# Loading the second weight strip of a fused attention and mixture kernel in eight 128 KB pieces over units 6 to 13, with its split on GpSimd in units 14 and 15

## The reference

```
scores = scale * q @ k^T           # 4 x 8 heads, 576 positions, head width 64
mask: 0 <= i - j < 64
attn = softmax(masked scores)      # then attn @ v -> x, 2304 tokens x 512
xn = x / sqrt(mean(x*x) + 1e-6) * rms_g
x  = silu(xn @ w_gate) * (xn @ w_val) @ w_out        # width 1536
e  = argmax(x @ moe2_w_gate)                         # 8 experts
out[token] = softmax(x @ moe2_w_gate)[e] * (relu(x @ w1[e]) @ w2[e])
```

## Time and profile before

| quantity | value |
|---|---|
| median of three runs | 817.53 us |
| profiled execution | 815.81 us |
| its span, first to last instruction | 814.0 us |
| TensorE (PE) busy | 802.3 us, 99% |
| VectorE (DVE) busy | 489.3 us, 60% |
| ScalarE (ACT) busy | 304.8 us, 37% |
| GpSimd (POOL) busy | 204.6 us, 25% |
| granted TensorE clock | 0.999 of full |

### The profile page before, as it was taken

One profiled execution on the slowest core, in us unless ns is written; L12 is line 12 of the kernel. 1 busy time (PEld: TensorE's weight loads), 2 busy tenths in 40 slices (PEclk: granted clock), 3 DMA queues, 4 the chain that ended last, 5 costly groups with the idle time before them and its releaser, 6 DMA issues.

```text
span 814.0 us, 15142 instructions
## 1 busy us (share of the span) xinstructions
PE 802.3 (99%) x4785; PEld 724.8 (89%) x4786; DVE 489.3 (60%) x999; ACT 304.8 (37%) x666; POOL 204.6 (25%) x183
## 2 busy tenths in 40 slices
PE   7999999999999999999999999999999999999996
PEld 7999999999999999999999999998888888888885
DVE  7888645667657764857586677727226445564252
ACT  7988742121321132131213124334324534543341
POOL 4596596031004000400220000052920110110100
PEclk9999999999999999999999999999999999999999
DMA  7997960020002002000200012226353643655100
GB/s 218 297 333 259 329 245 1 0 79 1 1 1 79 0 1 76 4 1 1 78 0 1 1 43 100 104 79 221 128 181 130 246 151 131 256 189 193 54 15 26
DMA packets 39809, 86.57 MB, mean 106 GB/s; under 512 B 4094, under 2 KB 13566, under 8 KB 39232
## 3 DMA queue, kind: packets, MB, share of 16 engines
q1 hardware_dynamic: 35568, 75.41, 26.9%
q0 software_dynamic: 3360, 10.23, 3.5%
q10 hardware_dynamic: 816, 0.12, 0.1%
HBM read 72.37 MB, written 14.16 MB: 106 GB/s over the span
## 4 chain that ended last, share of the span: by engine, by line
PE 96%; DMA 2%; issue 1%; SPq 0%; DVE 0%; ACT 0%; POOL 0%; POOLq 0%; ACTq 0%; DVEq 0%
PE ps L1085 28%; PE ps L1084 28%; PE ps L1083 28%; PE ps L1018 3%; PE ps L1230 2%; PE ps L1053 2%; PE ps L1038 1%; PE ps L1150 1%; PE ps L1012 1%; DMA vt<-vW 1%; DMA kt<-kT 0%; DMA qraw<-qT 0%; PE ps L1260 0%; DMA out<-osb,sidx 0%; PE ps L1268 0%
## 5 line engine op out<-in xcount | busy, mean ns | idle before, releaser
L1083 PE MATMUL ps<-xn_hi,GV_hi 128*128 128x384 f32 x576 | 194.1, 337 | 0.0
L1085 PE MATMUL ps<-xn_hi,GV_lo 128*128 128x384 f32 x576 | 193.3, 336 | 0.0
L1084 PE MATMUL ps<-xn_lo,GV_hi 128*128 128x384 f32 x576 | 192.9, 335 | 0.0
L1083 PEld LDWEIGHTS ps<-xn_hi,GV_hi 128*128 128x128 f32 x576 | 108.2, 188 | 2.8
L1084 PEld LDWEIGHTS ps<-xn_lo,GV_hi 128*128 128x128 f32 x576 | 108.2, 188 | 2.7
L1085 PEld LDWEIGHTS ps<-xn_hi,GV_lo 128*128 128x128 f32 x576 | 108.1, 188 | 0.0
L826 ACT ACTIVATE h_hi<-ps 128x384 fp32r<-128x384 f32 x72 | 35.5, 493 | 163.1 <-DVE ps L1446 161.4
L1476 DVE CUSTOM_DVE_ANT_0 ps<-ysb,wrb 128x512 f32<-128x512 f32 x120 | 92.3, 770 | 6.0 <-ACT ysb L833 1.0
L820 ACT ACTIVATE sig<-ps 128x384 f32<-128x384 f32 x71 | 35.0, 493 | 159.3 <-PE ps L1085 140.1
L1085 PE MATMUL ps<-Wo_hi,h_lo 128*128 128x512 f32 x216 | 85.5, 396 | 0.0
L1084 PE MATMUL ps<-Wo_lo,h_hi 128*128 128x512 f32 x216 | 85.3, 395 | 0.0
(11 more groups left out here) (183 smaller groups left out, 1407.9 us busy)
## 6 DMA issues: line engine op xcount, KB each, us to landing
EW_raw<-w SPq DMA_DIRECT2D x32, 1024.0 KB, 5.8
vt<-vW SPq DMA_DIRECT2D x16, 512.0 KB, 5.2
y_rows<-ysb SPq DMA_DIRECT2D x6, 768.0 KB, 4.1
kt<-kT SPq DMA_DIRECT2D x47, 96.0 KB, 4.6
qraw<-qT SPq DMA_DIRECT2D x15, 288.0 KB, 3.9
xraw<-xT_rows SPq DMA_DIRECT2D x5, 768.0 KB, 5.6
xT_rows<-xo SPq DMA_DIRECT2D x12, 288.0 KB, 3.6
raw_out<-w_out SPq DMA_DIRECT2D x3, 1024.0 KB, 7.9
```

The costliest lines, as they stand in the source:

```text
L1083: nc.tensor.matmul(out, a_hi, b_hi, start=start, stop=False)
L1084: nc.tensor.matmul(out, a_hi, b_lo, start=False, stop=False)
L1085: return nc.tensor.matmul(out, a_lo, b_hi, start=False, stop=stop)
```

## The change

Strip 0 is loaded as before, in units 2 to 5. The halves of strip 1 are each cut into two quarters of 128 KB (the rows of one of the two 128-row tiles in a half, 1 KB a partition), and one quarter is loaded in each of the units 6 to 13, gate in even, value in odd units. It stands in SyncE's queue at the place where the half stood. SyncE's two loops become unrolled code. GpSimd splits strip 1 after n = 14 and 15, and scales the first rows after n = 13.

```
-EARLY_HALVES = 4
+QUARTERS = 4
...
-            return 16 * (min(2 * c + 2, EARLY_HALVES) + max(c + 1 - EARLY_HALVES // 2, 0)) + 16
+            return 16 * ((2, 2 + QUARTERS)[min(c, 1)] + max(c - 1, 0)) + 16
...
-                sp.dma_start(GV_raw[:, bass.ds(h, 1), kind, :, :].rearrange("p a k f -> p (a k f)"),
-                             (w_gate, w_val)[kind][bass.ds(h, 1)].rearrange("a p f -> p (a f)")).then_inc(w_in[kind], 16)
+                sp.dma_start(GV_raw[:, h, kind, :, :].rearrange("p k f -> p (k f)"),
+                             (w_gate, w_val)[kind][h]).then_inc(w_in[kind], 16)
+
+            def load_quarter(i, kind):
+
+                h, k = 2 + i // 2, i % 2
+                sp.wait_ge(w_in[kind], 16 * (2 + i) + 16)
+                sp.dma_start(GV_raw[:, h, kind, k, :],
+                             (w_gate, w_val)[kind][h, :, k * STRIP:(k + 1) * STRIP]).then_inc(w_in[kind], 16)
...
+                if quarter is not None:
+                    load_quarter(quarter, u)
...
-            with sp.Fori(KEPT + 1, EARLY_HALVES + 1) as pair:
+            for i in range(QUARTERS - 1):
                 for u in range(2):
-                    unit(2 * pair + u, u, half=pair - 1)
-            with sp.Fori(EARLY_HALVES + 1, UNITS // 2 - 2) as pair:
-                for u in range(2):
-                    unit(2 * pair + u, u)
+                    unit(2 * (KEPT + 1 + i) + u, u, quarter=i)
             for u in range(2):
-                unit(UNITS - 4 + u, u, q=u == 0)
+                unit(UNITS - 4 + u, u, q=u == 0, quarter=QUARTERS - 1)
...
-            strip_at = {7: 0, 8: 1, 11: 2, 12: 3}
+            strip_at = {7: 0, 8: 1, 14: 2, 15: 3}
             square_at = {9: (0, 1), 10: (2, 3)}
-            scale_at = {14: range(KD)}
+            scale_at = {13: range(KD)}
```

More of the change, by code:

```diff
@@ L440, in _, with unit @@
             load_keys(3, 1)
-            def unit(n, u, q=True, k=True, half=None, store=store_xT):
+            def unit(n, u, q=True, k=True, half=None, quarter=None, store=store_xT):
                 store(n - 2, u)
```

## The result

The changed kernel takes 818.82 us, the median of 22 runs (816.04 to 820.87), against 817.31 us for the kernel before (22 runs, 815.63 to 818.71). The ratio is 1.002, interval 1.0011 to 1.0028: slower by 0.9 to 2.3 us; 0.2%, which I had set as the bound between no change and slower, is 1.64 us and lies within it. A second set of runs gave 1.0023 (1.0012 to 1.0033). The forecast was 818.6 us. Its closeness is partly luck: it was a change of +1.03 us on top of 817.53, the median of three runs, and the measured changes are +1.51 us on top of 817.31 and, in the second set, +1.79 on top of 817.36.

The account below looks back on a forecast made before the run. TensorE was taken as the bound, busy 802.3 of 814.0 us. The terms -0.72 + 0 + 1.48 + 0.27 = +1.03 us on the median 817.53 gave 818.6 us, 8-in-10 range 817.0 to 820.1.

Parts of the forecast that it names:

- Part 3: Split after unit 14's tile: waits for the last gate quarter, so TensorE waits 1.48 us for unit 15's tile.
- Part 4: Split after unit 15's tile: first dense rows' pieces come late, TensorE waits 0.14 and 0.13 us, cost 0.27 us.
- Part 1: Units 6 to 9: fewer weight bytes ahead of the values shorten TensorE's stalls, gain 0.72 us, range 0.3 to 0.88.
- Part 2: Units 10 to 13: added quarters find room on the DMA engines, cost 0, at most 0.37 us once.
- The sum: Whole kernel: relief, added bytes and both GpSimd waits together, +1.03 us, giving a median of 818.6 us.
- The fourth: TensorE's clock falls to half in the new gap before unit 15's mask, 1.6 us more, 820.2 us; chance 0.04.
- The first rival: Gate quarter's landing takes 5.8 us, TensorE waits 2.58 us for unit 15's tile, sum +2.35, 819.9 us; chance 0.20.
- the second: Gate quarter lands within 3.2 us, unit 15's tile is in time, only the gain is left, 816.8 us; chance 0.12.
- The third: Stalls of units 8, 9 and 12 stay and the wait for the tile is added, +1.75, 819.3 us; chance 0.10.

Follow-up runs that it names:

- run landed by unit 11: Changed kernel with the last gate and value quarters issued in units 10 and 11, none in units 12 and 13; ratio 0.9999, 816.51 us.
- gaps of chosen length: Kernel before with six, seven or eight needless squares on GpSimd delaying unit 15's tile; ratios 1.0002, 1.0025 and 1.0046.

## Why the prediction was right

**Part 3, the wait for unit 15's tile: right in mechanism and near in size.** Put at 1.48 us, it was 1.52 and 2.19 in the two traces. The closeness of the 1.52 is partly luck: there the landing was 0.5 us sooner than put, and the issue stood only 76.31 - 68.48 = 7.83 us ahead of TensorE's need. The landing was put at 4.7 us and was 4.2 and 4.9. In the first trace, besides the later landing, the issue came only 76.44 - 68.55 = 7.89 us ahead of TensorE's need, not the 77.17 - 68.96 = 8.21 taken from rows 6 and 9. The stall that I had counted as removed in unit 12 had delayed TensorE but not SyncE. I shifted everything together by it; not everything shifts. The run landed by unit 11 shows that the late landing is the cause.

**Part 4, the first rows: right.** Forecast 0.14 and 0.13. In the trace without a fall k = 0 is late by 5.09 - 4.91 = 0.18. In the one with the fall TensorE itself was so late that nothing waited (81.93 for the first piece's start, 85.06 for its use). Both splits behind unit 15's tile test it harder: 1.2 us expected, 1.19 measured.

**Part 1, the relief: right in sign, 0.1 us too large on average.** I took 0.72 from the one trace, 0.52 for units 9 to 12 and 0.20 ahead of them. Over all traces it is 0.48 and 0.13, together 0.61. In the two traces of the changed kernel the whole excess is 0.28 and 0.19 instead of 0.89, which looks like a hit and is better than the average. A stall of some tenths at a queue that is full moves from unit to unit between executions; the 5.16 of unit 11 in the first trace is one.

**Part 2, nothing for the bytes in units 10 to 13: mis-sized, but within its bound of 0.37.** The two traces of the changed kernel show nothing in units 13 and 14. The five with these loads together show 0.17 us on average, and up to 0.41.

**The sum.** The bare terms in the trace without a fall near 80 us end attention (its last L1059, at 90.68) 0.98 us later than before (89.70); I had +1.03. That trace has 0.4 us less excess than the average of its loads, so the bare cost is rather +1.4: over executions of mean clock 0.998 or more the median span is 815.5 (11) against 814.1 (21). The forecast of the change was thus about 0.4 us too small without any fall of the clock, and 0.5 to 0.8 with it.

**Rivals.** The fourth was the clock: I gave a fall behind the gap 0.04, priced at 1.6 us. The price was right (1.52). It came in one of the two traces of the changed kernel, so 0.04 was too small a chance. How often it comes the times can't say. Of the changed kernel's 34 executions 11 have a mean clock of 0.998 or more and a median span of 815.5 us, and 13 have spans of 817.8 or more (median 818.4), which is well over one fall of 1.6 us more; of the kernel before all but 2 of 64 are at 816.4 or less, against 814.1 for its own of 0.998 or more. Both traces of the changed kernel belong to those 13, and they differ: one has its second fall behind the gap, the other has it at 551 to 558 us, right behind the first. A mean clock of 0.995 or less (13 of 34 against 5 of 64) doesn't tell the two apart either: three traces without a gap have 0.995 and no fall near 80 us. What the clock adds to the bare +1.4 in the medians, 0.1 to 0.4 us, is therefore only in part the gap's, and how large a part is open. I had argued from the trace's short stalls, 0.5 us at most, which say nothing of a gap of 2 us. The gaps of chosen length say it. (With the rule of the Trainium skill, "TensorE: Matmul & The Clock Gate", Part 1, weighed there, that an idle engine drops to half clock, the two traces with a fall behind the gap agree; the falls near 554 us, where TensorE does not wait, it does not cover.) The first rival, a landing of 5.8 us, did not come (4.2 and 4.9), nor did the second: neither trace of the changed kernel has the tile in time. The third, that the stalls of units 8, 9 and 12 stay, came neither whole nor not at all: of 0.79 us in units 9 to 12 the traces with quarters keep 0.31 on average.

## What to carry to other kernels

Before work that waits for a transfer is put ahead of something urgent on an in-order engine, add up landing, work and the urgent item against the need; moving the same work behind the last urgent item costs nothing if the engine idles later. A load should be placed where the queue has room and its user where the engine has slack, and these two places have to be chosen together. Bytes that are moved along a full queue are partly paid for where they go: here 0.6 us was gained in all, and 0.17 given back in those that got them. And a prize of some tenths of a microsecond is to be read from several traces, since one trace gives it a place and a size that the next does not confirm.

## What the runs showed of the hardware

A wait of TensorE worth 2.2 us in the midst of dense work (busy before and after) was followed by 3.4 us at half clock, one worth 1.5 us in the same program was not (the trace names 1.95 and 1.28 us of them); with a gap of chosen length the trace shows it at a wait of 2.54 us and not at 0.73 and 1.64. Each of these is one trace.

The clock also falls where TensorE does not wait, behind or during 24 products with 8 columns that take 2.85 us, in half of the traces, at a cost of 1.6 us, once of 3.2. In the kernel before the executions part into two groups 1.6 us apart, so this fall is most likely the larger part of its spread of 3 us. Which execution gets it I could not tell from the traces.

Loads behind a full queue took much the same time, whatever their size: 4.2 and 4.9 us for 128 KB, 4.7 for 96 KB and 5.2 to 5.8 for 512 KB.
